# Linear attention and two mixtures on one core: range check split in two, opening reordered

## What is computed

```python
for t in range(S):
    state = alpha[:, :, t, :, None] * state + einsum('bhd,bhe->bhde', k[:, :, t], v[:, :, t])
    y[:, :, t] = einsum('bhd,bhde->bhe', q[:, :, t], state)
x = y.transpose(0, 2, 1, 3).reshape(1536, 384)
xn = x / sqrt(mean(x * x) + 1e-6) * rms_g
g = xn @ w_gate
x = (g * sigmoid(g) * (xn @ w_val)) @ w_out          # w_gate, w_val: 384 x 1536
p = probs / (probs.sum(-1) + 1e-9)
out = sum(p[:, e] * (relu(x @ w1[e]) @ w2[e]) for e in range(4))
```

## Time and profile before

| what | value |
|---|---|
| median of three runs | 694.67 us |
| the profiled execution's own time | 693.56 us |
| its span, first to last instruction | 691.8 us |
| PE busy | 681.8 us (99%) |
| DVE, ACT, POOL busy | 464.7, 266.0, 331.4 us |
| granted TensorE clock | 1.00 all through |

### The profile page before, as it was taken

The page is one execution under the profiler, slowest core; times in us unless marked ns, Lnnn a source line. Parts: engine busy times, 40 slices in busy tenths (PEclk is TensorE's granted clock), DMA queues, the critical chain, the costliest instruction groups (busy, mean ns, idle before and its releaser), DMA issues.

```text
span 691.8 us, 10697 instructions
## 1 busy us (share of the span) xinstructions
PE 681.8 (99%) x3973; PEld 632.0 (91%) x3973; DVE 464.7 (67%) x816; ACT 266.0 (38%) x484; POOL 331.4 (48%) x417
## 2 busy tenths in 40 slices
PE   7899999999999999999999999999999999999998
PEld 6699999999999999998999999999999999999997
DVE  6876657555465544217978777877787778767876
ACT  5823233223522243226534443444344434443430
POOL 5479661211111215773394577457745774577200
PEclk9999999999999999999999999999999999999999
DMA  8975380005102001000011110111011101100003
GB/s 185 226 166 127 78 166 0 9 1 113 25 4 75 1 2 46 1 0 24 1 46 47 46 45 1 46 46 46 1 46 46 47 1 46 46 24 1 23 1 136
DMA packets 72228, 34.53 MB, mean 50 GB/s; under 512 B 53872, under 2 KB 71664, under 8 KB 72176
## 3 DMA queue, kind: packets, MB, share of 16 engines
q1 hardware_dynamic: 71728, 33.85, 19.4%
q10 hardware_dynamic: 448, 0.00, 0.0%
HBM read 30.89 MB, written 2.36 MB: 48 GB/s over the span
## 4 chain that ended last, share of the span: by engine, by line
PE 95%; DVE 4%; issue 1%; ACT 0%; DVEq 0%
PE out_ps L1405 13%; PE out_ps L1407 13%; PE out_ps L1406 13%; PE hid_ps L1398 7%; PE hid_ps L1400 7%; PE hid_ps L1399 7%; PE at_ps L1646 5%; PE at_ps L1645 5%; PE at_ps L1644 4%; PE hid_ps L1645 2%; PE hid_ps L1646 2%; PE hid_ps L1644 2%; PE at_ps L1481 2%; PE at_ps L1495 2%; PE at_ps L1527 1%; PE out_ps L1645 1%
## 5 line engine op out<-in xcount | busy, mean ns | idle before, releaser
L1281 DVE SCALAR_TENSOR_TENSOR x<-out_ps,prob,x 128x384 f32<-128x384 f32 x180 | 110.2, 612 | 57.8 <-PE out_ps L1407 57.8
L1406 PE MATMUL out_ps<-early_r,late_r 128*128 128x384 f32 x384 | 129.4, 337 | 0.0
L1407 PE MATMUL out_ps<-early_r,late_r 128*128 128x384 f32 x384 | 129.3, 337 | 0.0
L1405 PE MATMUL out_ps<-early_r,late_r 128*128 128x384 f32 x384 | 129.0, 336 | 0.0
L699 POOL TENSOR_TENSOR hid_lo<-act_sb,hid_hi 128x384 fp32r<-128x384 f32 x44 | 44.9, 1019 | 162.3 <-ACT hid_hi L921 162.3
L971 ACT COPY late<-at_ps 128x512 f32<-128x512 f32 x105 | 61.8, 588 | 101.8 <-PE at_ps L1646 98.7
L1247 DVE TENSOR_TENSOR act_sb<-hid_ps,act_sb 128x384 f32<-128x384 f32 x48 | 26.6, 554 | 80.1 <-PE hid_ps L1400 80.1
L1405 PEld LDWEIGHTS out_ps<-early_r,late_r 128*128 128x128 f32 x384 | 72.1, 188 | 6.1 <-DVE x L1281 0.2
L1406 PEld LDWEIGHTS out_ps<-early_r,late_r 128*128 128x128 f32 x384 | 72.0, 188 | 5.6
L1407 PEld LDWEIGHTS out_ps<-early_r,late_r 128*128 128x128 f32 x384 | 72.1, 188 | 0.0
L921 ACT CAST hid_hi<-act_sb 128x384 fp32r<-128x384 f32 x48 | 24.6, 513 | 107.9 <-DVE act_sb L1247 107.9
(11 more groups left out here) (291 smaller groups left out, 1619.3 us busy)
## 6 DMA issues: line engine op xcount, KB each, us to landing
stage<-in_moe_w_dram SPq DMA_DIRECT2D x32, 384.0 KB, 3.4
stage<-in_moe_w_out_dram SPq DMA_DIRECT2D x4, 576.0 KB, 4.6
out_dram<-x SPq DMA_DIRECT2D x12, 192.0 KB, 1.9
alpha_all<-in_alpha_dram SPq DMA_DIRECT2D x6, 288.0 KB, 4.5
stage<-in_moe_w_gate_dram SPq DMA_DIRECT2D x8, 216.0 KB, 3.7
stage<-in_moe_w_val_dram SPq DMA_DIRECT2D x8, 216.0 KB, 4.0
a_tm<-in_alpha_dram SPq DMA_DIRECT2D x9, 192.0 KB, 4.0
k_tm<-in_k_dram SPq DMA_DIRECT2D x9, 192.0 KB, 4.3
```

The source lines that it names most:

```text
L1281: dve.scalar_tensor_tensor(out=a, in0=part, scalar=p, in1=a, op0=ALU.mult, op1=ALU.add).then_inc(s_acc, 1)
L1405: pe.matmul(dst, ah, bh, start=first, stop=False)
L1406: pe.matmul(dst, ah, bl, start=False, stop=False)
L1407: return pe.matmul(dst, al, bh, start=False, stop=last)
```

## The change

Six things change.

1. The flag is taken twice. W 0 now covers only E 0 and E 1. A second W and ND (`W 1`, `ND 1`) stand at place 24 of the first mixture, and cover all eight parts. DVE, ACT (at N of quarter 1) and SP read a flag again there. PE's SS of quarter 1 waits for it.
2. E 2 to E 7 leave the opening and stand in the first mixture, at places 11, 13, 14, 19, 20 and 21.
3. Their transfers leave SP's early queue. Three follow weight piece 5, and three follow piece 8. The second three wait until five checks are done (three buffers in `x2` are used in turn).
4. SP reads the second flag ahead of `prob` and of all transfers for quarters 2 and 3.
5. The opening has a new order: Y 0 before TK 2, KV 2 and ST 2 before S 3, W 0 before Y 2. The last chunk's states of pairs 2 and 3 become a step of their own (`CA 2`, `CA 3`) behind XS and SS, ahead of R.
6. In the branch that isn't taken, blocks of 16 steps take the place of 24.

```diff
-        alpha_all = sb("alpha_all", [P, APARTS, AW], stack=reg_w)
+        half_range = sb("half_range", [P, 2, AW], stack=reg_w)
+        ROUND = 3
+        part_range = x2[:, 0:ROUND * AW].rearrange("p (n x) -> p n x", n=ROUND)
...
-                                            "M 1", "E 0", "S 0", "KS 0", "E 1", "C 1", "S 1", "KS 1", "E 2", "T 2",
-                                            "KV 0", "ST 0", "KV 1", "E 3", "T 3", "ST 1", "E 4", "TK 2", "TQ 2",
-                                            "Y 0", "TK 3", "TQ 3", "E 5", "M 2", "M 3", "Y 1", "S 2", "KS 2",
-                                            "S 3", "KS 3", "E 6", "E 7", "KV 2", "ST 2", "KV 3", "ST 3", "Y 2",
-                                            "W 0", "SQ 1", "SQ 2", "ND 0", "YD 3", "SQD 3", "N 0", "XS 0", "SS 0", "R 0"))]
+                                            "M 1", "E 0", "S 0", "KS 0", "E 1", "C 1", "S 1", "KS 1", "T 2",
+                                            "KV 0", "ST 0", "KV 1", "T 3", "Y 0", "ST 1", "TK 2", "TQ 2",
+                                            "TK 3", "TQ 3", "Y 1", "M 2", "M 3", "S 2", "KS 2", "KV 2",
+                                            "ST 2", "S 3", "KS 3", "KV 3", "W 0", "Y 2", "ST 3",
+                                            "SQ 1", "SQ 2", "ND 0", "YD 3", "SQD 3", "N 0", "XS 0", "SS 0", "CA 2",
+                                            "CA 3", "R 0"))]
+        RANGE_AT = (11, 13, 14, 19, 20, 21)
...
+                        if i == 0 and 3 * f + sub == STEP * NP:
+                            yield "W", 1, 0
+                            yield "ND", 1, 0
...
+                        if i == 0 and 3 * f + sub in RANGE_AT:
+                            yield "E", 0, 2 + RANGE_AT.index(3 * f + sub)
...
+                c, home = CHECKED[n], part_range[:, (n - 2) % ROUND, :]
+                if n == 2:
+                    sp.wait_ge(s_y, NP)
+                    sp.wait_ge(s_st, NCH * NP)
+                elif n == 2 + ROUND:
+                    sp.wait_ge(s_exc, 2 + ROUND)
...
                 load_piece(n)
+                if n == 5 or n == 8:
+                    for c in range(ROUND):
+                        load_alphas((2 if n == 5 else 2 + ROUND) + c)
+            sp.wait_ge(s_wild, 2)
+            with sp.If(sp.value_load(wild[0:1, 2:3])):
+                serve_steps()
             sp.dma_start(prob[:, :, :], probs.rearrange("(t p) e -> p t e", p=P)).then_inc(s_prob, 16)
...
-                elif name == "N" and i == 0:
-                    act.wait_ge(s_wild, 1)
-                    is_wild = act.value_load(wild[0:1, 0:1])
+                elif name == "N" and i < 2:
+                    act.wait_ge(s_wild, i + 1)
+                    is_wild = act.value_load(wild[0:1, i:i + 1])
...
+                        if i == 1:
+                            pe.wait_ge(s_wild, 2)
```

More of the change, by code:

```diff
@@ L22 @@
 MID, HALF = 0.95, 0.25
-TB = 24
+TB = 16
 OCT = 8
@@ L219, in gated_attention_two_moe @@
         assert spare_at[0] <= NQ * KT * TQ - TQ
+        ROUND = 3
+        part_range = x2[:, 0:ROUND * AW].rearrange("p (n x) -> p n x", n=ROUND)
+        assert ROUND * AW <= NQ * KT * TQ - TQ and APARTS == 2 + 2 * ROUND
         prob_flat = prob[:, :, :].rearrange("p t e -> p (t e)")
@@ L267, in gated_attention_two_moe @@
         s_hole = sem("s_hole")
-        s_sq_redo = sem("s_sq_redo")
+        s_sq_redo = [sem(f"s_sq_redo{i}") for i in range(NQ)]
         s_sq, s_sqsum, s_ss, s_rms = sem("s_sq"), sem("s_sqsum"), sem("s_ss"), sem("s_rms")
@@ L298, in gated_attention_two_moe @@
         s_slow_turn = sem("s_slow_turn")
-        s_redo = sem("s_redo")
+        s_redo = [sem(f"s_redo{i}") for i in range(NQ)]
         def heads(t, rows=R):
@@ L562, in _ @@
                     sp.sem_inc(s_slow_turn, 1)
+            for which in (0, 1, 2, 3):
+                load_quarter(0, which, H // 2, H, s_half[which])
+            load_quarter(0, 0, 0, H // 2)
+            load_quarter(0, 1, 0, H // 2)
+            load_quarter(0, 2, 0, H // 2)
+            load_quarter(0, 3, 0, H // 2)
+            load_piece(0)
+            load_piece(1)
+            fill_holes(0)
+            next_a(1)
+            load_piece(2)
+            next_kq(1)
+            load_piece(3)
+            sp.wait_ge(s_wild, 1)
+            with sp.If(sp.value_load(wild[0:1, 0:1])):
+                serve_steps()
             next_v(1)
@@ L811, in check_range @@
             def check_range(c):
-                part = alpha_all[:, (CHECKED[c] - 2) % APARTS, :]
+                part = half_range[:, c, :] if c < 2 else part_range[:, (c - 2) % ROUND, :]
                 if c == 0:
@@ L1154, in _ @@
                     kv = banks[2][:, 0:NCH * 2 * D].rearrange("p (c x) -> p c x", c=NCH)
-                    for c in range(NCH):
+                    for c in range(NCH - 1 if i == 0 and f >= NP - 2 else NCH):
                         if c == NCH - 1 and i % QB == QB - 1:
@@ L1166, in _ @@
                             op0=ALU.mult, op1=ALU.mult).then_inc(s_st, 1)
-                        dve.wait_ge(s_st, NCH * u + c + 1)
+                        dve.wait_ge(s_st, states_before(i, f) + c + 1)
+                elif name == "CA":
+                    dec, banks = own_of(i, f)[0], own_of(i, f)[5]
+                    total = heads(banks[2][:, (NCH - 1) * 2 * D:NCH * 2 * D])
+                    own(dve.tensor_tensor(total, total, state_blocks(st_in(i, f, NCH - 1)[0:R, :]), ALU.add))
+                    own_done()
+                    dve.scalar_tensor_tensor(
+                        out=state_blocks(st_out(i, f, NCH - 1)[0:R, :]), in0=total,
+                        scalar=dec[0:R, NCH * CH - 1:NCH * CH], in1=heads(own_head),
+                        op0=ALU.mult, op1=ALU.mult).then_inc(s_st, 1)
                 elif name == "YD":
@@ L1179, in _ @@
                 elif name == "W":
-                        dve.wait_ge(s_exsum, 1)
-                        own(dve.tensor_reduce(excess_sum[:, :], at_ps[0][0:1, 0:APARTS], mybir.AxisListType.X, ALU.add))
-                        own_done()
-                        dve.tensor_scalar(wild[:, :], excess_sum[:, :], 0.0, 0.0, ALU.is_le, ALU.is_equal
-                                          ).then_inc(s_wild, 1)
+                    dve.wait_ge(s_exsum, i + 1)
+                    own(dve.tensor_reduce(excess_sum[:, :], excess_rows(i), mybir.AxisListType.X, ALU.add))
+                    own_done()
+                    if i == 0:
+                        own(dve.tensor_scalar(first_fits[:, :], excess_sum[:, :], 0.0, None, ALU.is_le))
+                    else:
+                        own(dve.tensor_scalar(wild[:, 2:3], excess_sum[:, :], 0.0, first_fits[:, 0:1], ALU.is_le,
+                                              ALU.is_lt))
+                    dve.tensor_scalar(wild[:, i:i + 1], excess_sum[:, :], 0.0, 0.0, ALU.is_le, ALU.is_equal
+                                      ).then_inc(s_wild, 1)
                 elif name == "ND":
-                    dve.wait_ge(s_wild, 1)
-                    with dve.If(dve.value_load(wild[0:1, 0:1])):
+                    own_done()
+                    dve.wait_ge(s_wild, i + 1)
+                    with dve.If(dve.value_load(wild[0:1, 2 * i:2 * i + 1])):
                         attention_by_steps()
```

59 lines of the change are left out of this document (22 added, 37 removed).

## The result

The changed kernel took 699.34 us (median of four runs, 698.75 to 700.44), the kernel before 694.86 us beside it. The ratio is 1.0068, with a 95% interval of 1.0051 to 1.0086: slower by 4.5 us in the medians. On another occasion the same two gave 698.8 and 694.8 us, ratio 1.0059 (1.0042 to 1.0076). The forecast was 698.7 us, between 696.3 and 701.5.

What follows compares the result with a forecast made beforehand. PE was taken to bound the first mixture and DVE the opening. Opening +0.1, mixture checks +3.35 and second flag +0.6 make +4.05 us; on 694.67 this forecasts 698.7 us, range 696.3 to 701.5.

Steps and rivals of the forecast that it cites:

- What bounds the kernel: PE, fully busy from 46 to 110 us, bounds the first mixture, so its waits lengthen the span; DVE bounds the opening.
- The opening: Up to DVE's gate product: earlier copies and shorter square against carried states ahead of the root; +0.1 us, between -1.0 and +0.6.
- E 2: Check in the first mixture behind pair 1's k_sm, where ACT then idles about 4 us; costs nothing.
- E 3 and E 4: Checks ahead of a silu on ACT in the mixture; delay cast and k_sm, so PE waits 1.15 us.
- E 5 to E 7: Later mixture checks, two ahead of a silu and one behind it; cast and k_sm 3.25 us late, PE waits 2.2 us.
- Second group of transfers: Held on SP, delaying weight piece 9 and hid_lo in the mixture; 0 us, covered by PE's wait before k_sm.
- Second flag: SP's read delays quarter 2's factors, DVE's clamp and the last output product; +0.6 us, between 0 and 2.8.
- fourth rival: Late weight piece 9 or quarter 2's factors, k and q cost 2.2 to 5 us more, 700.9 to 704 us; chance 0.12.
- the first (the checks fall into gaps): Mixture checks fit ACT's real gaps and only the opening counts: 694.8 us, or up to 1.4 us more; chance 0.10.
- the second (faster): The opening's gain is kept and DVE's clamp of quarter 1's factors is shorter: -1.8 us, 692.9 us; chance 0.05.
- the third: Only part of the mixture checks' waits reaches PE: +1.4 to +2.9 us, 696.1 to 697.6 us; chance 0.15.
- the main term: The checks on ACT in the first mixture make PE wait for k_sm of pairs 2 and 3; together +3.35 us.

Runs made afterwards that it cites:

- both: Changed kernel with the six later checks at places 10, 11, 12, 17, 18, 23 and quarter 2's first transfers ahead of SP's second flag read; 694.64 us, ratio 0.9994.
- places: Changed kernel with only the six later checks moved, to places 10, 11, 12, 17, 18 and 23; 695.7 us, ratio 1.0011 to the kernel before.
- best: The kernel both with pair 2's carried state moved ahead of DVE's read of the first flag; 693.87 us, ratio 0.9994 to the kernel before.
- best_aligned: The kernel best with the new one-element tile put into the tile of excess_sum, restoring the old addresses; 693.07 us, ratio 0.9979 to the kernel before.

## Why the prediction was right

The forecast was 4.05 us over before by steps, the traces show 5.4 and 5.0 us, and the medians 4.5 and 4.0 us. The sum goes by a trace of before whose execution was shorter than the median; the second trace has a span 0.5 us longer, and against it the two differences are 4.9 and 4.5 us.

- **What bounds the kernel.** PE in the mixture, as read: each us for which it waited is in the span, and from 115 us on nothing changed (the shift is 5.43 us there and 5.4 us at the end).
- **The opening, forecast +0.1, measured +0.43 and +0.89** (against the second trace of before -0.03 and +0.43). The upper end of +0.6 was added up wrongly: with the square not shortened and the readout not earlier, its own terms give 1.15 - 0.1 = +1.05 us, and the measured 0.89 lies between the two. By parts: the square's 0.2 us was right against the first trace; in the second the square took 1.28 us, so there it was worth 0.7. The carried states cost 1.06 us ahead of the root, where I had 1.3; less the 0.15 us of idle that is 0.91 against 1.15. The 0.1 us of slack behind the root isn't there: from the root to the gate product it is 1.87 us before and 1.85 after. The readout ended later than I forecast, and this is the step that failed. The copies were to start at 30.3 and start at 30.80. I had moved instructions only, and took for granted that quarter 0's inputs arrive as before. The new tile shifted them by 32 bytes, and the return to the old address is worth 0.42 us at the same place. By estimate, without it the copies would start at 30.4 (30.80 less 0.42) and the first gate product at 37.35, level with the first trace of before. In the first trace, the one with the fall of the clock, all this came another 0.46 us later.
- **E 2**: nothing, as forecast.
- **E 3 and E 4, forecast 1.15, measured 1.05 us.** Less the opening's 0.89 us, the silu came 2.81 us late (77.70 against 74.00; 2.95 forecast) and the cast 2.08 us (78.83 against 75.86; 2.25 forecast).
- **E 5 to E 7, forecast 2.2, measured 1.95 us.** Here the third check stands behind the silu and sets the cast (94.98 us), as worked out.
- **Second group of transfers, forecast 0 (covered), measured 0.** A wait of 0.35 us for `hid_lo` appeared in one of two traces of the kernel, and it came out of the wait for `k_sm` (1.30 us beside it, 1.70 without it, the same rest).
- **Second flag, forecast +0.6, measured 1.1 us** (`both` against `places`), some 0.5 us more than my value and well inside its bounds of 0 to 2.8. The factors left SP at 100.42, as forecast (100.5). But their issue took 2.52 us, not 1.92, and the clamp started 3.67 us behind the last issue, where I had a landing of 3.0, so at 106.61 and not near 105. How much of these two durations is the shifted address, no run here isolates. The sum had a slip besides: 102.4 + 3.0 is 105.4 and not 105, and with it the term is +1.0 us. And the slack was mis-sized the other way. DVE stood 3.07 us before the clamp, not 1.8, and only 1.1 us of it reached the end: some 2.0 us were covered, where I had 1.2. So that the term came within 0.5 us is partly luck. A part of the 1.1 us did not go over the clamp: quarter 2's k and q, issued behind the factors until 110.31 us, put off PE's transposes of q (114.62 us, 0.57 behind those of k, against 0.33 before) by 0.24 us. The prediction had this in its fourth rival alone.
- **W 1 on PE**, which I had not priced: its products, and a readout that starts behind them. In `both`, where nothing else is left, the rest is 0.2 us longer than before. In the changed kernel about 0.4 us lies between the state product of pair 3 and the last output product that the transfers don't explain.

Of the rivals, the first (the checks fall into gaps) is refuted by the two waits for `k_sm`, the second (faster) by the sign, and the third by the size of both waits. The fourth was right in its kind, as the late transfers did cost more, but by 0.5 us, less than the 2.2 it named. The mechanism of the main term, 3.0 of the 5.4 us, was read right. That the medians came out 0.6 and 0.1 us from the forecast, and the spans 1.3 and 0.9 us over the 695.9 forecast, owes something to errors that partly cancel: -0.35 us on the checks, +0.3 to +0.8 on the opening, +0.5 on the flag, +0.2 to +0.4 on W 1.

## What to carry to other kernels

An engine that is idle two thirds of the time can still hold up the one that is full. Find the idle stretch in its rows by time and put the added work at its start, behind what others wait for: the same six checks cost 3.2 us where they stood and nothing measurable a few places on or back. A read of a flag on the queue that issues transfers delays all transfers behind it (here 1.1 us of the whole), so issue those first that don't depend on it. And look at the addresses after a change that adds a tile, however small: compare the landings of the same transfers between the two traces before blaming the queue.

## What the runs showed of the hardware

**Transfers of short rows depend on the address in the SBUF.** These are rows of 192 bytes. Landing of `q_tm` in the first 60 us, shortest and median: 2.7/2.9, 2.6/3.0, 2.5/2.7 and 2.5/2.6 us in the four traces with `q_tm` at 45632, and 3.2 to 3.4 and 3.6 to 3.9 us in the ten with it at 45664. The DMA engines' busy share (before the last number) tells the same. From 8 to 10 us, `best` and then `best_aligned`:

```profile
8.00:10.00 2.00, 1.54 (x14) 1.54 (x15) 1.80 (x5) 1.94 (x5) 0.01 (x1) 1.00 1.21 180
```

```profile
8.00:10.00 2.00, 2.00 (x19) 2.00 (x19) 1.80 (x5) 1.94 (x5) 0.00 (x0) 1.00 0.95 175
```

At about the same GB/s the engines are busy 1.21 in one and 0.95 in the other: each packet takes longer. Which boundary counts is not isolated. 45632 is a multiple of 64 and 45664 only one of 32. But the heads' rows of `q_tm`, `k_tm` and `a_tm` start 256 bytes apart. At 45632 each ends just at a multiple of 256, and at 45664 each runs 32 bytes over it. (The Trainium skill, DMA: Bandwidth & Descriptors, section "How a descriptor splits into AXI transactions", splits reads at multiples of 256 bytes, which would give each of these rows a second transaction if it held for writes too. The same page's figures would make this 9 beats instead of 8; the share here rose by 27%, or 24% per GB/s, so that count alone doesn't give the size. Its page Collectives: The Full Stack, section "🎯 Rules for kernel authors", asks for buffers on 32 bytes. Both of these addresses are, and they differ.) `v_tm` speaks for the 64 bytes. Its rows start 192 bytes apart, so at its old address (64064) all start at a multiple of 64, and yet half of them run over a multiple of 256. In `best_aligned` it lands in 2.4/2.7 us, as `q_tm` does, whose rows cross none; in `best` in 3.2/3.7 us. So crossing 256 bytes does not by itself make a row slow. That a multiple of 64 is what counts fits all four tiles, but no run tries other addresses.

**The clock in the opening.** In five of the ten traces with the shifted address the granted clock fell to 0.50 (1.2 GHz) for some 3 to 7 us between 8 and 22 us, each time during or right after an idle of PE of 0.9 to 1.4 us (before `q_tm` in three of them, before POOL's `a_first` in two), and in none of the four with the old one. Without a fall PE had idled just as long in others (1.02 us in the second trace of the changed kernel, 1.00 us in the second of before). The two traces of the changed kernel, one with the fall and one without, differ by 0.46 us at the end of the opening. Single executions of the kernel before had mean clocks of 0.995 to 1.00 as well, so the fall is not peculiar to the change. No run here isolates its cause.
